# Up-projection tiles in pairs, with 64-row matmuls for the last term

## The reference

```python
w = softmax(weight, axis=-1)                    # 8 heads x 7 taps
x = causal_conv(x, w)                           # 7 taps along the sequence, a filter for each head
x = (sigmoid(x @ w_gate) * (x @ w_val)) @ w_out # 192 -> 1536 -> 192
h = x @ w_in                                    # 192 -> 2048
P = a[0] + a[1]*h + a[2]*h*h + a[3]*h*h*h
Q = 1.0 + abs(b[0])*abs(h) + abs(b[1])*h*h
out = (P / (Q + 1e-6)) @ w_out2                 # 2048 -> 192
```

## Time and profile before

| | |
|---|---|
| median of 3 runs | 1335.96 us (1335.45 to 1337.26) |
| profiled execution, its own time | 1335.3 us |
| span of its trace | 1333.5 us |
| PE, DVE, ACT, POOL busy | 96%, 94%, 83%, 49% of the span |
| weight loads busy | 77% of the span |
| one chunk of the loop | 79.8 us |

### The profile page before, as it was taken

The page is one execution under the profiler, slowest core; times in us unless marked ns, Lnnn a source line. Parts: engine busy times, 40 slices in busy tenths (PEclk is TensorE's granted clock), DMA queues, the critical chain, the costliest instruction groups (busy, mean ns, idle before and its releaser), DMA issues.

```text
span 1333.5 us, 16870 instructions
## 1 busy us (share of the span) xinstructions
PE 1279.1 (96%) x5440; PEld 1023.5 (77%) x5440; DVE 1252.3 (94%) x1201; ACT 1104.9 (83%) x1278; POOL 658.5 (49%) x337
## 2 busy tenths in 40 slices
PE   5989999999999999999999999999999999999876
PEld 4768887787878778787787878778787787888654
DVE  7789999999999999999999999999999999998898
ACT  6588898888888888898888888888897988888674
POOL 1426455454446456455455445456455555554432
PEclk9999999999999999999999999999999999999888
DMA  8000000010100000000000100000000000000000
GB/s 223 23 0 21 1 13 21 9 24 0 32 0 12 20 8 24 0 14 18 10 21 0 32 0 12 20 8 24 0 17 14 12 20 0 20 0 13 1 12 12
DMA packets 15960, 23.66 MB, mean 18 GB/s; under 512 B 2240, under 2 KB 10048, under 8 KB 15936
## 3 DMA queue, kind: packets, MB, share of 16 engines
q1 hardware_dynamic: 14160, 21.30, 5.9%
q10 hardware_dynamic: 1776, 2.06, 0.7%
HBM read 13.13 MB, written 6.29 MB: 15 GB/s over the span
## 4 chain that ended last, share of the span: by engine, by line
PE 86%; DVE 8%; issue 3%; ACT 1%; POOL 0%; DMA 0%; DVEq 0%; ACTq 0%; SPq 0%
PE up_ps L303 10%; PE up_ps L304 10%; PE up_ps L305 10%; PE up_ps L307 10%; PE up_ps L306 10%; PE acc_main L310 7%; PE acc_main L313 7%; PE acc_main L311 7%; PE acc_tail L314 7%; PE acc_tail L312 7%; DVE tail_twice L1109 1%; DVE denom L1189 1%; DVE numer L1152 1%; DVE numer L1160 1%; DVE denom L1179 1%
## 5 line engine op out<-in xcount | busy, mean ns | idle before, releaser
L971 POOL TENSOR_TENSOR frac_low<-denom,seed 128x1024 fp32r<-128x1024 f32 x126 | 377.2, 2993 | 551.1 <-DVE denom L1189 549.0
L962 POOL TENSOR_TENSOR gated_low<-gated,gated_high 128x512 fp32r<-128x512 f32 x192 | 264.2, 1392 | 109.7 <-ACT gated_high L657 109.4
L303 PE MATMUL up_ps<-x_high,up_high 128*128 128x512 f32 x640 | 256.8, 401 | 39.7 <-DVE x_low L1221 16.4
L304 PE MATMUL up_ps<-x_high,up_low 128*128 128x512 f32 x640 | 251.7, 393 | 0.0
L305 PE MATMUL up_ps<-x_low,up_high 128*128 128x512 f32 x640 | 251.7, 393 | 0.0
L307 PE MATMUL up_ps<-x_tail_low,up_tail 128*128 128x512 f32 x640 | 250.7, 392 | 0.0
L306 PE MATMUL up_ps<-x_tail_high,up_tail 128*128 128x512 f32 x640 | 250.5, 391 | 0.0
L677 ACT ACTIVATE numer<-up_ps,coef 128x1024 f32<-128x1024 f32 x128 | 153.9, 1202 | 38.2 <-PE up_ps L307 35.7
L303 PEld LDWEIGHTS up_ps<-x_high,up_high 128*128 128x128 f32 x640 | 120.9, 189 | 80.1 <-DVE denom L1142 19.7
L1152 DVE TENSOR_TENSOR numer<-up_ps,numer 128x1024 f32<-128x1024 f32 x128 | 156.3, 1221 | 25.8 <-ACT seed L668 18.7
L668 ACT ACTIVATE seed<-up_ps,coef 128x1024 f32<-128x1024 f32 x128 | 142.2, 1111 | 44.4 <-PE up_ps L307 28.2
(11 more groups left out here) (86 smaller groups left out, 2279.7 us busy)
## 6 DMA issues: line engine op xcount, KB each, us to landing
x_raw<-x_chunks SPq DMA_DIRECT2D x16, 393.0 KB, 3.2
out_chunks<-out_main SPq DMA_DIRECT2D x16, 256.0 KB, 2.1
tail_twice<-conv SPq DMA_DIRECT2D x60, 64.0 KB, 2.0
out_chunks<-tail_part SPq DMA_DIRECT2D x16, 128.0 KB, 2.3
numer<-w_out SPq DMA_DIRECT2D x1, 1536.0 KB, 9.7
seed<-w_out ACTq DMA_DIRECT2D x1, 1152.0 KB, 12.0
denom<-w_in SPq DMA_DIRECT2D x2, 512.0 KB, 4.8
denom<-w_gate SPq DMA_DIRECT2D x1, 576.0 KB, 5.7
```

The lines of the kernel that those rows point to most:

```text
L303: nc.tensor.matmul(acc, up_high[:, cols], x["high"][:], start=True, stop=False)
L304: nc.tensor.matmul(acc, up_low[:, cols], x["high"][:], start=False, stop=False)
L962: nc.gpsimd.tensor_tensor(gated_low[:, b], gated[:, b], gated_high[:, b], ALU.subtract).then_inc(gated_low_done, 1)
L971: nc.gpsimd.tensor_tensor(ring(frac_low, j, 2, LOW_RING), ring(denom, j), ring(seed, j), ALU.mult).then_inc(frac_low_done, 1)
```

## The change

Up tiles are done two at a time (`up_pair`): a gate tile and the value tile of the same number, or two h tiles. Each of the two has its four full matmuls as before; then come, one behind the other, the two matmuls for x's low tail part, each with 64 rows: that of the first tile on partitions 0 to 63, that of the second on 64 to 127. They write different banks. The product of low by low is no longer computed. For this the high part of the tail's weights has to be on the upper half of the partitions for first tiles and on the lower half for second tiles, so the value weights and the second half of `w_in` have their halves exchanged in `up_tail`, and h tile n is paired with tile n + 8 (`pair_tiles`) instead of n + 1; the order in which the second block's `down` runs over its weights follows. Gate and value tiles alternate over the banks. The order of every engine's list is new, in the start, the loop and the end; the loop body holds the same calls as before, in other places, and begins at another point of the chunk.

```diff
-GATE_PLACES = (4, 5, 6)
-VAL_PLACES = (7, 8, 9)
+GATE_PLACES = (4, 6, 8)
+VAL_PLACES = (5, 7, 9)
...
+        def pair_tiles(j):
+
+            return j // 2, j // 2 + pairs2
...
-            return (raw[:, start:end], raw[0:tail, cols + start:cols + end],
+            halves = slice(0, tail), slice(tail, P)
+            high, low = halves if (name, n) in (("gate", 0), ("gate", 1), ("in", 0)) else halves[::-1]
+            return (raw[:, start:end], raw[high, cols + start:cols + end], high, low,
                     slice(first_col[name] + start, first_col[name] + end))
...
-            def up(i, w, place, col, x):
-                reader, count = bank_reader(i, w, place)
-                if reader is not None:
-                    after(pe, reader, count)
-                acc, cols = up_bank(i, w, place), slice(col, col + P)
-                nc.tensor.matmul(acc, up_high[:, cols], x["high"][:], start=True, stop=False)
-                nc.tensor.matmul(acc, up_low[:, cols], x["high"][:], start=False, stop=False)
-                nc.tensor.matmul(acc, up_high[:, cols], x["low"][:], start=False, stop=False)
-                nc.tensor.matmul(acc, up_tail[:, cols], x["tail_high"][:], start=False, stop=False)
-                return nc.tensor.matmul(acc, up_tail[:, cols], x["tail_low"][:], start=False, stop=True)
+            def up_pair(i, w, place, cols, x):
+
+                accs = [up_bank(i, w, place + a) for a in range(2)]
+                for a in range(2):
+                    reader, count = bank_reader(i, w, place + a)
+                    if reader is not None:
+                        after(pe, reader, count)
+                    nc.tensor.matmul(accs[a], up_high[:, cols[a]], x["high"][:], start=True, stop=False)
+                    nc.tensor.matmul(accs[a], up_low[:, cols[a]], x["high"][:], start=False, stop=False)
+                    nc.tensor.matmul(accs[a], up_high[:, cols[a]], x["low"][:], start=False, stop=False)
+                    nc.tensor.matmul(accs[a], up_tail[:, cols[a]], x["tail_high"][:], start=False, stop=False)
+                return [nc.tensor.matmul(accs[a], up_tail[rows, cols[a]], x["tail_low"][rows], start=False, stop=True)
+                        for a, rows in enumerate((slice(0, tail), slice(tail, P)))]
...
+                    cols = [slice(first + k * P, first + (k + 1) * P) for first in (0, d_ff1)]
+                    gate_tile, val_tile = up_pair(i, w, GATE_PLACES[b], cols, x0)
+                    gate_tile.then_inc(gate_ready, 1)
+                    val_tile.then_inc(val_ready, 1)
```

More of the change, by code:

```diff
@@ L339, in down_fraction @@
                         after(pe, out_tail_summed, i - 1)
-                    for a in range(2):
-                        down(acc2_main, acc2_tail, down2[:, j + a], ring(frac_high, j + a, 1, HIGH_RING),
+                    for a, n in enumerate(pair_tiles(j)):
+                        down(acc2_main, acc2_tail, down2[:, n], ring(frac_high, j + a, 1, HIGH_RING),
                              ring(frac_low, j + a, 1, LOW_RING),
@@ L448, in _ @@
[L448 to L464, removed]
@@ L531, in _ @@
             down_gated(chunks - 1, 3, 2)
+            down_fraction(*late(-6))
             down_fraction(*late(-5))
@@ L1384, in chunk @@
-                split_x0_tail(i + 1)
-                quadratic(i + 1, 0, 0)
-                high_fraction(i, 3, 1)
-                cubic(i + 1, 0, 0)
-                quadratic(i + 1, 0, 1)
-            chunk_loop(dve, chunk)
-            denominator(*late(-2))
-            product(*late(-4))
+            chunk_loop(dve, chunk)
+            gate(chunks - 1, 2, 0)
+            sum_out_tail(chunks - 1)
+            gate(chunks - 1, 2, 1)
+            product(*late(-7))
+            rest(*late(-7))
@@ new lines, in _ @@
+            gate(chunks - 1, 2, 2)
+            quadratic(*late(-4))
+            high_fraction(*late(-6))
+            cubic(*late(-4))
+            quadratic(*late(-3))
+            cubic(*late(-3))
+            denominator(*late(-4))
+            denominator(*late(-3))
+            product(*late(-6))
+            rest(*late(-6))
+            gate(chunks - 1, 3, 0)
+            gate(chunks - 1, 3, 1)
+            high_fraction(*late(-5))
+            product(*late(-5))
+            rest(*late(-5))
@@ L1395, in _ @@
+            high_fraction(*late(-4))
+            gate(chunks - 1, 3, 2)
+            quadratic(*late(-2))
+            cubic(*late(-2))
+            product(*late(-4))
+            quadratic(*late(-1))
+            denominator(*late(-2))
+            high_fraction(*late(-3))
+            rest(*late(-4))
+            product(*late(-3))
+            split_x1_main(chunks)
+            sum_x1_tail(chunks)
             cubic(*late(-1))
-            rest(*late(-4))
-            denominator(*late(-1))
@@ L1422, in _ @@
             cubic(*late(3))
-            high_fraction(*late(1))
+            product(*late(1))
             denominator(*late(3))
-            product(*late(1))
+            rest(*late(1))
             high_fraction(*late(2))
-            rest(*late(1))
+            sum_out_tail(chunks)
             quadratic(*late(4))
-            sum_out_tail(chunks)
             cubic(*late(4))
@@ L1453, in _ @@
             product(*late(6))
+            rest(*late(6))
             high_fraction(*late(7))
-            rest(*late(6))
             last_low(*late(6))
```

569 lines of the change are left out of this document (260 added, 309 removed).

## The result

The changed kernel takes 1423.39 us (median of 4 runs, 1422.47 to 1423.71) against 1335.93 us before, a ratio of 1.065 (95% interval 1.063 to 1.067). It is slower by 87 us, where 1305 us was forecast and the range ended at 1345.

A forecast was written before the change was run, and what follows sets the result against it. PE was taken to bound the loop at 79.8 us a chunk, DVE close behind. Savings of 24 us in the loop, 3 and 2.5 around it and 1.5 at the start, together 31, gave 1305 us, range 1288 to 1345.

The forecast's parts named there:

- I take a saving of 0.07 to 0.226 us: Pair's last slot on PE: two 64-row matmuls side by side save this much, 1.5 to 4.5 us a chunk.
- under the one matmul ahead of them: Pair's last slot: both halves' weight loads, 0.22 us together, fit under the preceding matmul, so nothing is lost.
- its other end: Pair's worst cases at shape changes: from a gain of 0.02 us to losses of 0.10 or 0.48 us a pair.
- the handover: Between a chunk's two blocks: PE loses about 0.8 us, DVE waits 1.8 us, in a chain starting at ACT's sigmoid(i, 0, 0).
- Half matmuls cost more than they save: Rival: PE empties at each change between 128 and 64 rows; 1340, 1367 or up to 1490 us, chance 0.20.
- the drain's side: The view that changing the tiling mode drains PE, making half matmuls a loss; chance 0.20.
- PE now has up to 3 us slack a chunk to run ahead: Loop: with pairs holding two banks each, PE can still run ahead and keep DVE fed.
- 1.3 us of idle time: Loop: DVE's idle time a chunk falls to this from 3.3 us, giving a chunk of 77.8 us.
- its 76.5 us a chunk stay: Loop: DVE's busy time is unchanged because the loop body has the same calls on it.
- PE as the bound before: Loop of the old kernel: PE's matmuls take 78.1 of 79.8 us a chunk, DVE 3.3 us behind.
- the end: Last 98.5 us of the kernel: DVE sets the pace there, so the change saves 0.
- DVE is the next bound at some 77.8 us: Loop: once PE is relieved DVE sets the pace, a chunk 2.0 us shorter than 79.8; chance 0.60.

The follow-up runs named there:

- the stream: A separate kernel of matmuls alone, without waits, in repeated groups of 128-row and 64-row matmuls; 8 full and two opposite halves took 2.47 us.
- b_nine: Kernel before, old orders, copy_x1_part ahead of sigmoid(i, 0, 0), fifth matmul of gate and first h tiles left out: 1307.43 us, ratio 0.979.
- a_nine: Changed kernel with nine full matmuls a pair, no 64-row ones, the first tile's fifth left out: 1338.1 us, ratio 1.002.
- b_short: Kernel before with six of seven convolution steps on a third of their columns, so less DVE work: 1334.49 us.
- b_copy_first: Kernel before with one line moved on ACT, copy_x1_part(i) ahead of sigmoid(i, 0, 0): 1320.9 us, ratio 0.989.
- a_full_each: Changed kernel with 128 rows in all ten matmuls of a pair, each tile's fifth right behind its fourth: 1372.17 us, ratio 1.027.

## Why the prediction was wrong

The step that failed is the first term, "I take a saving of 0.07 to 0.226 us" a pair. Measured, a pair loses 0.21 us (2.47 against 2.26), which is 4.2 us a chunk where 1.5 to 4.5 were to be gained. The forecast took it that the halves' loads fit "under the one matmul ahead of them". The two loads do start together, but not ahead: at a change of shape they start with their own matmul, and the three starts around the change come 0.10, 0.20 and 0.11 us later than within a shape (0.32, 0.43 and 0.34 against 0.226). The prediction named these mechanisms for its other end: an emptied PE, an exposed load, and a second full matmul that is late as behind the gap at the handover, there by 0.10 us. Its prices for a pair there ran from a gain of 0.02 us over a loss of 0.10 to one of 0.48; 0.21 lies between. The rival "Half matmuls cost more than they save", with its threshold of 0.113 us a change, is what happened: the measured price is 0.21 us a change. The drain that the Trainium skill states ("TensorEngine Tiling (Array Packing)", Key Properties) fits these prices, as each change of shape costs time here, but no trace shows PE empty at one. Its other rule, that row tiles on different rows run at the same time ("TensorE: Matmul & The Clock Gate", Part 3), the trace bears out: in the stream L89 and L90 both start at 64.81 us. The forecast gave the drain's side a chance of 0.20.

The second step that failed is "PE now has up to 3 us slack a chunk to run ahead", with the sum built on it, DVE's 76.5 us of work and 1.3 us of idle time. No row showed the new orders. It was right of the old ones: b_nine has 77.8 us a chunk and DVE idle 1.4 us. In the new ones with the same nine slots (a_nine) DVE's idle time is 1.4 us too, but "its 76.5 us a chunk stay" is not so, as it is busy 78.5; and cutting DVE's work by 2.4 us brought nothing, so the length of a_nine's chunk doesn't follow DVE's work. PE's slack is lost in the first 36.5 us of that chunk, where PE waits, and is missing in the other 43.4, where it is full. That DVE's work could grow was not considered, only that it could shrink.

The three parts of the miss, from 1305 to 1423 us, are then: 2 us to b_nine (1307), 31 us for the new orders (a_nine, 1338) and 85 us for what a pair costs above nine slots (1423). By the pair's price it would be 20 x (2.47 - 2.04) = 8.6 us a chunk, of which 5.3 show; the rest falls where PE waited anyway.

Right were: PE as the bound before, by the spacing of its matmuls (b_short); the end, but for 1.2 us; the two halves side by side; and the handover, that ACT's list and not a matmul began the chain, whose waits of DVE and PE are gone in the changed kernel. Its worth was taken as 0.8 us of the chunk; b_copy_first brought 1.15 us, 15 us in all. That DVE is the next bound at some 77.8 us is borne out in its number by b_nine, but no run took work off DVE there; a_nine, where DVE is busier still and not the bound, shows that a high busy share doesn't prove it. The forecast of 1305 us is thus met by b_nine, a kernel in other orders that leaves a term out, and this agreement shows the mechanism only in part.

Open stays which calls of the new lists hold a_nine at 79.9 us. With ten matmuls a pair the late first tile is part of it (a_full_each); DVE's load is not, and two `denominator` calls placed sooner made it worse. ACT's list with its `square` calls placed sooner was not tried.

## What to carry to other kernels

Before a matmul of another shape is put into a dense stream, price the way out and back: here 0.42 us for a visit, nearly two slots of 512 columns, so that two concurrent pairs break even and by the estimate above three are needed for a gain. A slot saved on the bound is worth little once another engine is close behind (4.5 us less work on PE brought 0.8 us a chunk in b_nine), and orders made anew for it are a change with a price of its own: try the saving in the old orders first, by leaving work out. When a chain begins at an engine's place in its own list, moving one line may be worth more than the rebuild.

## What the runs showed of the hardware

Two 64-row matmuls on opposite partitions start within 0.01 us of each other and together take no longer than one full one (0.227 us a pair alone in the stream). A visit to the 64-row shape between 128-row matmuls costs 0.41 to 0.45 us above its slots, whether one, two or four half matmuls are made in it (2.44, 2.47 and 4.52 us against 9, 9 and 18 slots of 0.226). Weight loads, which run one matmul ahead within a shape (load at 703.27 us, matmul at 703.50), are not made ahead across a change of shape (load and matmul both at 703.82, and both at 704.25).
